# The attention of the first 256 tokens rebuilt, value matmuls with 64-column weights, and three weight groups split by VectorE and GpSimd

## The chip, the cores and the metric

One core of one Trainium2 chip runs the kernel. The metric is the device time of one execution in microseconds (us), as the median of several runs. TensorE does the matmuls, VectorE (DVE), ScalarE (ACT) and GpSimd (POOL) the element-wise work, and SyncE (SP) issues every transfer.

## The reference, cut to what matters

An attention with a window and sinks over 2 sequences of 768 tokens, 8 heads of 64, followed by two dense layers on the 1536 tokens (512 features in, 2048 inside, 512 out), all in float32:

```python
scores = scale * np.matmul(q, k.transpose(0, 1, 3, 2))
is_sink = pos[None, :] < n_sink                 # n_sink = 4
in_window = (rel >= 0) & (rel < window)         # window = 128
scores = np.where(is_sink | in_window, scores, -1e9)
a = softmax(scores)                             # max, exp, sum + 1e-9, divide
x = np.matmul(a, v)                             # heads side by side: 512 features
h = x @ w_in;  g = 0, h or (h + 1)**2 / 4       # first layer, by h <= -1, h >= 1, between
x = g @ w_out
h = x @ w_in2; g = h if h > 0 else exp(h) - 1   # second layer
y = g @ w_out2
```

## The kernel before, in words

Tokens are taken in six chunks of 256 (`NC = 6`). Activations lie with features on the partitions. For each chunk the attention gives `x` (4 tiles of 128 features, one for each pair of heads), and the first layer runs 16 steps `t` over the 2048 inner features: `hidden` (L457) makes 128 of them in 12 matmuls, `outward` (L474) adds the part of step `t-2` to the output in 12 more. The second layer runs over chunks of 512 tokens.

Precision: the layers' matmuls take operands in a rounded 32-bit form (fp32r), and each product is made of three matmuls (high by high, low by high, high by low), so every operand is split into a high part (a rounding copy on ACT) and a low part (source minus high on DVE). Weights come in 32 groups of 128x1024 (16 of each layer), through raw buffers, and are split once (`split_weights`, L581 on ACT, L757 on DVE).

The attention of chunk `c+1` is interleaved with the first layer of chunk `c` (the plan `BESIDE`); the attention of chunk 0 has nothing beside it and runs alone in front (`ALONE`). For one head: `split_head` (q and k into parts), `scores` (four fp32r matmuls of 260 columns, L414 and L415: 256 keys of the window and 4 sinks, for each of two blocks of 128 queries), `maxima` (a fused mask, scale and maximum in DVE, L716), `exponent` (ACT, L544), `normalise` (DVE, L724 to L730), `transposes` (TensorE, L426), the copy of the transposed probabilities (ACT, L550). For a pair of heads: `values`, whose weights have 128 columns of which 64 are zeros for either head (`vs` is 3*HD wide with zeros in it), so that both heads add into one bank of 128 partitions; these are plain float32 matmuls, each of which the trace shows as two records (L447 to L449), and one matmul for the sinks (L454). `write_x` and `split_x` then make `x`, `x_hi`, `x_lo`.

In chunk 0 the same steps run head by head with doubled buffers (banks of the layers, corners of `xy` and `wout_*`). Five weight groups (`EARLY = 5`, plan `SPLITS_ALONE`) are split by ACT and DVE inside this stretch; the other 11 of the first layer are split in chunk 0's layer, group `5+t` at step `t`. The layers start when `x_lo` of the first pairs and groups 0 and 1 are there. GpSimd only builds masks and copies the mask of each chunk (L402). SP issues all loads in one written-out order, waiting in it for buffers.

The order on every engine is written out by hand; engines meet only at semaphores.

Of the kernel before, what the change touches and what calls it, by code (L numbers as in the profile page):

```python
# [54 lines left out]
SPLITS_ALONE = {6: [0], 7: [1], 8: [2], 9: [3, 4]}  # L55
EARLY = sum(map(len, SPLITS_ALONE.values()))

# [3 lines left out]
def attention_plan(head_at, by_halves):  # L61

    scores, exps, transposes, values = ([[] for _ in range(head_at[-1] + 4)] for _ in range(4))
    for h, at in enumerate(head_at):
        scores[at].append(h)
        exps[at + 1].append(h)
        transposes[at + 2].append(h)  # L70
        if by_halves and h < HEADS - 2:
            values[at + 4].append((h // 2, [h % 2]))
        elif h % 2 == 1:
            values[at + 3].append((h // 2, [0, 1]))
    return scores, exps, transposes, values


ALONE = attention_plan(list(range(HEADS)), True)
BESIDE = attention_plan([2, 3, 5, 6, 8, 9, 11, 12], False)


def build(nc, q_t, k_t, v_w, v_s, w_in, w_out, ident_d, out, n_sink, window):
# [8 lines left out]
    with ExitStack() as ctx:  # L91
# [16 lines left out]
        small = sb("small", [P, 4 * QB + 1])  # L108
        top, total = (small[:, n:n + 2 * QB].rearrange("p (h j) -> p h j", h=2) for n in (0, 2 * QB))
        half = small[:, 4 * QB:4 * QB + 1]  # L110
# [14 lines left out]
        vs = sb0("vs", [P, 2, 3, 3 * HD])  # L125
        vsink = sb0("vsink", [P, 2, P])
# [19 lines left out]
        waited_act, waited_dve = sem("waited_act"), sem("waited_dve")  # L146
        qk_loaded = [sem(f"qk_loaded{n}") for n in range(4)]
# [33 lines left out]
        def tiles(parts, first, count, width):  # L181
            return parts[:, first:first + count, :].rearrange("p f m -> p (f m)")[:, 0:width]

        heads_at_once = [(k_hi[:, :], k_lo[:, :], q_parts[:, :], s_ps, t_ps),
                         (tiles(wout_hi, FT - 2, 2, QB * SW), tiles(wout_lo, FT - 2, 2, QB * SW),
                          tiles(wout_hi, FT - 3, 1, CT), h_ps, y_ps[0])]
        pairs_at_once = [(probs[:, :, :], (probs_t[:, 0, :], probs_t[:, 1, :]), xy[:, 2, 0:CT], o_ps),
                         (xy[:, 3, CT:CT + QB * 2 * SW].rearrange("p (j n) -> p j n", j=QB),
                          tuple(b[:, :, :].rearrange("p s t -> p (s t)") for b in (ramp, g_full)),
                          xy[:, 0, CT:2 * CT], y_ps[1])]  # L190
        pair_beside = (*pairs_at_once[0][:2], sinks_t[:, :], o_ps)
        loaded_heads = [(ks[:, s, :], qs[:, s, :]) for s in range(2)]
        loaded_heads += [(xy[:, 2, CT + s * QB * SW:CT + (s + 1) * QB * SW], q)
                         for s, q in enumerate((xy[:, 1, CT:2 * CT], xy[:, 3, 0:CT]))]

        def is_first(c):
            return isinstance(c, int) and c == 0

        assert CT + 2 * QB * SW <= TOK and QB * SW <= 2 * DM

        def head_work(c, h):

            return heads_at_once[h % 2 if is_first(c) else 0]

        def pair_work(c, p):


            return pairs_at_once[p % 2] if is_first(c) else pair_beside

        def loaded_head(c, h):  # L210
            return loaded_heads[h % 4 if is_first(c) else h % 2]

        def heads_before(c, h):
            return h - 1 if is_first(c) else c * HEADS + h

        def pairs_before(c, p):
            return p - 1 if is_first(c) else c * PAIRS + p
# [10 lines left out]
        FEW = RAW - 2  # L230
# [45 lines left out]

        block = ctx.enter_context(nc.Block())
# [3 lines left out]
        def _(sp):  # L281
            def load_head(c, h):

                if not is_first(c):
                    sp.wait_ge(qk_lo_ready, c * HEADS + (h - 1))
                elif h >= 4:
                    sp.wait_ge(qk_lo_ready, h - 3)
                for to, src in zip(loaded_head(c, h), (k_t, q_t)):
                    sp.dma_start(to, src[bass.ds(c * HEADS + h, 1)].rearrange("o p n -> (o p) n")).then_inc(qk_loaded[h % 4], 16)

            def load_values(c, p):
                s = p % 2
                if not is_first(c) or p >= 2:
                    sp.wait_ge(attn_ready, c * PAIRS + (p - 1))
                n = c * PAIRS + p
# [9 lines left out]
            def load_weights(i):  # L305
                n = order[i]
                layer, m = n // NW, n % NW
                if splits_until_free(i) > 0:
                    sp.wait_ge(w_lo_ready, splits_until_free(i))
                if i < NW and place[i] >= FEW:  # L310
                    sp.wait_ge(x_written, PAIRS)
                if i >= NW:
                    sp.wait_ge(attn_ready, NC * PAIRS)
# [3 lines left out]
            load_head(0, 0)  # L317
            load_head(0, 1)
            load_head(0, 2)
            sp.dma_start(ident[:, :], ident_d).then_inc(ident_loaded, 16)  # L320
            load_head(0, 3)
            load_head(0, 4)
            load_values(0, 0)
            load_weights(0)
            load_head(0, 5)
            load_head(0, 6)
# [566 lines left out]
```

## Time and profile before

| | |
|---|---|
| median of 3 runs | 666.1 us (665.94 to 667.99) |
| the profiled execution | 667.29 us, its span 665.3 us |
| TensorE matmuls busy | 642.4 us, 97% of the span |
| DVE, ACT, GpSimd busy | 390.8, 361.6, 9.4 us |
| first matmul of the layers | at 38.69 us of the span |
| second layer starts | at about 399 us |

The span runs from the first to the last instruction. The profiled execution took 2.0 us more than its span and 1.2 us more than the median of the runs.

### The profile page before, as it was taken

What the parts mean: (1) busy time and instruction counts of PE and PEld (TensorE: products, weight loads), DVE (VectorE), ACT (ScalarE), POOL (GpSimd) and SP (SyncE); (2) the same over time, 40 slices, a digit from 0 to 9 for tenths busy, and PEclk for the clock granted to TensorE, in tenths of its full rate; (3) what the DMA queues carried; (4) which work ended last, traced back from release to release, by engine and by line L of the source; (5) the groups of instructions that cost most, each with busy time, mean ns of one, the idle gap of its engine ahead of it and who ended that gap; (6) DMA issues with size and microseconds to landing.
All of it is one profiled execution on the core that took longest, in us unless ns stands there. A gap on an engine that the chain in (4) does not pass through costs nothing.

```text
span 665.3 us, 12399 instructions
## 1 busy us (share of the span) xinstructions
PE 642.4 (97%) x4204; PEld 582.4 (88%) x4204; DVE 390.8 (59%) x1022; ACT 361.6 (54%) x854; POOL 9.4 (1%) x28
## 2 busy tenths in 40 slices
PE   3888999999999999999999999999999999999998
PEld 3778999999999999999999998888888888888886
DVE  6989986886788588868866884322332222322221
ACT  6887766665665565656656665333453333533333
POOL 3000000000000000000000000000000000000000
PEclk9999999999999999999999999999999999999999
DMA  8477320431233023204205530000010000100001
GB/s 276 155 253 276 95 70 25 113 87 51 68 92 96 25 82 109 71 24 112 68 0 191 191 127 1 1 0 1 1 63 0 0 0 0 63 0 0 0 0 64
DMA packets 25805, 47.39 MB, mean 71 GB/s; under 512 B 2929, under 2 KB 10929, under 8 KB 25777
## 3 DMA queue, kind: packets, MB, share of 16 engines
q1 hardware_dynamic: 25776, 47.03, 22.7%
q8 instruction: 16, 0.26, 0.2%
q14 instruction: 13, 0.10, 0.0%
HBM read 43.88 MB, written 3.15 MB: 71 GB/s over the span
## 4 chain that ended last, share of the span: by engine, by line
PE 85%; DVE 11%; issue 2%; ACT 1%; DMA 1%; SPq 0%; ACTq 0%; DVEq 0%
PE h_ps L469 12%; PE h_ps L471 12%; PE h_ps L470 12%; PE y_ps L484 9%; PE y_ps L486 9%; PE y_ps L485 9%; PE s_ps L486 3%; PE s_ps L485 3%; PE s_ps L484 3%; PE o_ps L447 2%; PE t_ps L426 2%; PE s_ps L414 1%; DVE wout_lo L762 1%; PE s_ps L415 1%; PE o_ps L449 1%
## 5 line engine op out<-in xcount | busy, mean ns | idle before, releaser
L469 PE MATMUL h_ps<-x_hi,win_hi 128*128 128x256 f32 (+1 forms) x576 | 184.5, 320 | 1.3 <-DVE x_lo L769 0.5
L471 PE MATMUL h_ps<-x_hi,win_lo 128*128 128x256 f32 (+1 forms) x576 | 182.7, 317 | 0.0
L470 PE MATMUL h_ps<-x_lo,win_hi 128*128 128x256 f32 (+1 forms) x576 | 182.3, 316 | 0.0
L484 PE MATMUL y_ps<-g_hi,wout_hi 128*128 128x256 f32 (+1 forms) x480 | 145.2, 302 | 1.5 <-DVE g_lo L775 1.3
L486 PE MATMUL y_ps<-g_hi,wout_lo 128*128 128x256 f32 (+1 forms) x480 | 144.9, 302 | 0.0
L485 PE MATMUL y_ps<-g_lo,wout_hi 128*128 128x256 f32 (+1 forms) x480 | 144.6, 301 | 0.0
L792 DVE SCALAR_TENSOR_TENSOR g_full<-g_full,h_ps 128x512 f32<-128x512 f32 x48 | 33.0, 688 | 151.8 <-ACT g_full L622 151.8
L469 PEld LDWEIGHTS h_ps<-x_hi,win_hi 128*128 128x128 f32 x576 | 108.1, 188 | 11.1 <-DVE g_full L788 1.1
L470 PEld LDWEIGHTS h_ps<-x_lo,win_hi 128*128 128x128 f32 x576 | 108.2, 188 | 8.4
L471 PEld LDWEIGHTS h_ps<-x_hi,win_lo 128*128 128x128 f32 x576 | 108.2, 188 | 7.2
L775 DVE TENSOR_TENSOR g_lo<-g_full,g_hi 128x256 fp32r<-128x256 f32 (+1 forms) x144 | 73.6, 511 | 53.5 <-ACT g_hi L609 52.9
L609 ACT CAST g_hi<-g_full 128x256 fp32r<-128x256 f32 (+1 forms) x144 | 68.5, 476 | 66.7 <-DVE g_full L792 34.1
L484 PEld LDWEIGHTS y_ps<-g_hi,wout_hi 128*128 128x128 f32 x480 | 90.1, 188 | 7.2 <-issue 1.7
L485 PEld LDWEIGHTS y_ps<-g_lo,wout_hi 128*128 128x128 f32 x480 | 90.1, 188 | 4.2
L486 PEld LDWEIGHTS y_ps<-g_hi,wout_lo 128*128 128x128 f32 x480 | 90.1, 188 | 3.6
L620 ACT ACTIVATE ramp<-h_ps 128x512 f32<-128x512 f32 x48 | 28.8, 599 | 117.4 <-PE h_ps L471 116.8
L544 ACT ACTIVATE probs<-s_ps,small 128x260 f32<-128x260 f32 x84 | 39.2, 470 | 22.9 <-DVE small L719 22.9
L617 ACT ACTIVATE ramp<-h_ps,small 128x256 f32<-128x256 f32 x96 | 45.5, 474 | 5.7 <-PE h_ps L471 5.5
L786 DVE SCALAR_TENSOR_TENSOR g_full<-ramp 128x256 f32<-128x256 f32 x96 | 40.3, 420 | 8.8 <-ACT ramp L617 8.7
L788 DVE TENSOR_TENSOR g_full<-g_full,h_ps 128x256 f32<-128x256 f32 x96 | 40.4, 421 | 3.3
L550 ACT COPY probs_t<-t_ps 128x512 f32<-128x512 f32 x42 | 24.7, 588 | 24.8 <-PE t_ps L426 24.8
L486 PE MATMUL s_ps<-g_hi,wout_lo 128*128 128x512 f32 x96 | 37.8, 394 | 0.0
(122 smaller groups left out, 862.7 us busy)
## 6 DMA issues: line engine op xcount, KB each, us to landing
ks<-in_k SPq DMA_DIRECT2D x44, 260.0 KB, 2.7
vs<-in_v SPq DMA_DIRECT2D x24, 288.0 KB
qs<-in_q SPq DMA_DIRECT2D x44, 128.0 KB, 2.6
raw<-in_w_in SPq DMA_DIRECT2D x11, 512.0 KB, 4.6
raw<-in_w_out SPq DMA_DIRECT2D x11, 512.0 KB, 4.4
out_y<-xy SPq DMA_DIRECT2D x12, 256.0 KB, 2.1
xy<-in_w_in SPq DMA_DIRECT2D x5, 512.0 KB, 5.8
xy<-in_w_out SPq DMA_DIRECT2D x5, 512.0 KB, 6.3
```

What stands on the lines that cost most here:

```text
L469: pe.matmul(o, win_hi[:, k, f], x_hi[:, k, :], start=(k == 0), stop=False)
L470: pe.matmul(o, win_hi[:, k, f], x_lo[:, k, :], start=False, stop=False)
L471: last = pe.matmul(o, win_lo[:, k, f], x_hi[:, k, :], start=False, stop=(k == KT - 1))
L484: pe.matmul(o, wout_hi[:, t, cols], g_hi[:, t % GR, :], start=begin, stop=False, skip_group_check=True)
L485: pe.matmul(o, wout_hi[:, t, cols], g_lo[:, t % GR, :], start=False, stop=False, skip_group_check=True)
L486: last = pe.matmul(o, wout_lo[:, t, cols], g_hi[:, t % GR, :], start=False, stop=(t == FT - 1), skip_group_check=True)
L544: nc.scalar.activation(probs[:, j, hh * SW:(hh + 1) * SW], banks[j][:, 0:SW], ACT.Exp, bias=top[:, hh, j:j + 1], accum_out=total[:, hh, j: ...
L609: nc.scalar.copy(g_hi[:, t % GR, :], g_full[:, t % 2, :]).then_inc(g_hi_ready, 1)
L617: nc.scalar.activation(ramp[:, t % 2, :], h, ACT.Relu, bias=half[:, 0:1], scale=0.5).then_inc(ramp_ready, 1)
L775: nc.vector.tensor_tensor(g_lo[:, t % GR, :], g_full[:, t % 2, :], g_hi[:, t % GR, :].bitcast(F32), ALU.subtract).then_inc(g_lo_ready, 1)
L786: nc.vector.scalar_tensor_tensor(g, r, 1.0, r, ALU.min, ALU.mult).then_inc(bent_ready, 1)
L788: nc.vector.tensor_tensor(g, g, h, ALU.max).then_inc(g_ready, 1)
```

## The change

1. **The attention of chunk 0** is rewritten pair by pair, two pairs in flight. Query block 0 sees only its own 128 keys and block 1 sees 256 (`SEEN_OF`, 384 probabilities for a head instead of 520); sinks are inside the window there, so their columns, transposes and matmuls go. Scores are plain float32 matmuls on the 64 partitions of a head, with no split of q and k. Four maxima are followed by one negation for the pair, and one addition and one reciprocal serve four rows of sums. `x_hi` and `x_lo` are made from the bank (`x` itself is not written). q, k and v of the chunk have arrays of their own.
2. **The value matmuls of every chunk** take 64 weight columns and write the 64 partitions of their head; the two heads alternate. `vs` is 2*HD wide, without zeros.
3. **Three weight groups** (`EARLY = 3` instead of 5) are split ahead of the layers, by a copy on DVE and a subtraction on GpSimd; the remaining 13 are split at steps 0 to 12 of chunk 0 (`splits_first`). GpSimd's mask copy for chunk 1 stands behind its subtractions. `FEW` is 5 instead of 4, and the loads are issued in another order.

```diff
-SPLITS_ALONE = {6: [0], 7: [1], 8: [2], 9: [3, 4]}
-EARLY = sum(map(len, SPLITS_ALONE.values()))
+EARLY = 3
+SEEN = P + WIN
+SEEN_OF = (slice(0, P), slice(P, SEEN))
+KEYS_OF = (slice(0, P), slice(0, WIN))
+IN_FLIGHT = 2
-        FEW = RAW - 2
+        FEW = RAW - 1
...
# SyncE
+            load_first_head_pair(0)
+            load_first_head_pair(1)
+            sp.dma_start(ident[:, :], ident_d).then_inc(ident_loaded, 16)
+            load_first_values(0)
+            load_first_head_pair(2)
+            load_first_values(1)
+            load_weights(0)
+            load_first_head_pair(3)
+            load_first_values(2)
+            load_first_values(3)
+            load_weights(1)
             load_weights(2)
             load_weights(3)
             load_weights(4)
             load_head(1, 0)
+            load_head(1, 1)
+            load_values(1, 0)
             load_weights(5)
             load_weights(6)
+            load_head(1, 2)
             load_weights(7)
             load_weights(8)
             load_head(1, 3)
             load_values(1, 1)
+            load_weights(9)
...
# GpSimd
+            for i in range(EARLY):
+                hi, lo = w_parts(order[i])
+                pool.wait_ge(first_w_hi, i + 1)
+                nc.gpsimd.tensor_tensor(lo, split_source(i), hi.bitcast(F32), ALU.subtract).then_inc(first_w_lo, 1)
+            pool.wait_ge(first_max, HEADS * QB)
+            nc.gpsimd.tensor_copy(mask[:, :], masks[:, 1, :]).then_inc(mask_ready, 1)
...
# TensorE
+            def first_scores_of(p):
+                pe.wait_ge(first_qk_loaded[p], 32)
+                (q, k), banks = first_qk[p], flight[p % IN_FLIGHT][0]
+                if p >= IN_FLIGHT:
+                    pe.wait_ge(first_exp, (p - IN_FLIGHT + 1) * 2 * QB)
+                for j in range(QB):
+                    for hh in range(2):
+                        dims = slice(HD * hh, HD * (hh + 1))
+                        last = pe.matmul(banks[hh][:, SEEN_OF[j]], q[dims, j * P:(j + 1) * P], k[dims, KEYS_OF[j]], ...)
+                last.then_inc(first_scores, 1)
+            def first_transposes(p):
+                if p > 0:
+                    pe.wait_ge(first_copied, 2 * p)
+                for hh in range(2):
+                    pe.wait_ge(first_probs, (2 * p + hh + 1) * QB)
+                    for n in range(3):
+                        last = pe.transpose(h_ps[hh][:, n * P:(n + 1) * P], seen_probs(p, hh)[:, n * P:(n + 1) * P], ident[:, :])
+                    last.then_inc(first_probs_t, 1)
+            def first_values(p):
+                pe.wait_ge(first_v_loaded[p], 16)
+                pe.wait_ge(first_copied, 2 * (p + 1))
+                if p >= IN_FLIGHT:
+                    pe.wait_ge(x_lo_ready, p - IN_FLIGHT + 1)
+                for block, queries, keys_t in ((0, slice(0, CT), slice(0, CT)), (1, slice(P, CT), slice(CT, CT + P))):
+                    for hh in range(2):
+                        last = pe.matmul(o_bank[dims, queries], first_v[p][:, block * P + HD * hh:...], probs_t[hh][:, keys_t], ...)
+                last.then_inc(first_attn, 1)
...
-                for hh in halves:
-                    v, pt = vs[:, s, :, HD * hh:HD * hh + P], probs_t[hh]
-                    pe.matmul(o_bank[:, 0:CT], v[:, 1, :], pt[:, P:P + CT], ...)
-                    pe.matmul(o_bank[:, 0:P], v[:, 0, :], pt[:, 0:P], ...)
-                    pe.matmul(o_bank[:, P:CT], v[:, 2, :], pt[:, P + CT:P + CT + P], ...)
+                for block, queries, keys_t in ((1, slice(0, CT), slice(P, P + CT)), (0, slice(0, P), slice(0, P)),
+                                               (2, slice(P, CT), slice(P + CT, 2 * CT))):
+                    for hh in range(2):
+                        dims = slice(HD * hh, HD * (hh + 1))
+                        pe.matmul(o_ps[dims, queries], vs[:, s, block, dims], probs_t[:, hh, keys_t], ...)
...
+            first_scores_of(0)
+            first_scores_of(1)
+            first_scores_of(2)
+            pe.wait_ge(ident_loaded, 16)
+            first_transposes(0)
+            first_scores_of(3)
+            first_values(0)
+            for p in range(1, PAIRS):
+                first_transposes(p)
+                first_values(p)
...
# ScalarE: four exponents a pair, two copies of 384 columns a pair, one copy for x_hi
+            first_exponents(0)
+            first_exponents(1)
+            for p in range(PAIRS):
+                first_copies(p)
+                if p + IN_FLIGHT < PAIRS:
+                    first_exponents(p + IN_FLIGHT)
+                first_x(p)
...
# VectorE
+            def first_weights_hi(i):
+                dve.wait_ge(raw_loaded[place[i]], 16 * raw_count(i))
+                nc.vector.tensor_copy(w_parts(order[i])[0], split_source(i)).then_inc(first_w_hi, 1)
...
+            first_maxima(0)
+            first_maxima(1)
+            first_normalise(0)
+            first_maxima(2)
+            first_normalise(1)
+            first_maxima(3)
+            first_x(0)
+            first_normalise(2)
+            first_weights_hi(0)
+            first_x(1)
+            first_weights_hi(1)
+            first_normalise(3)
+            first_x(2)
+            first_weights_hi(2)
+            first_x(3)
```

`first_maxima`, `first_normalise` and `first_x` on DVE hold, for a pair: four fused maxima (128, 256, 128, 256 columns) and one negation; one addition, one reciprocal and four multiplications; one subtraction from the bank.

## Rows read from the trace of the kernel before

**Rows 1.** Page: the chain that ended last, by engine.
```profile
PE 85%; DVE 11%; issue 2%; ACT 1%; DMA 1%; SPq 0%; ACTq 0%; DVEq 0%
```
**Rows 2.** Windows by stage: us, busy of each engine, clock, DMA share, GB/s.
```profile
0.00:38.70 38.70, 25.50 (x129) 20.29 (x129) 30.10 (x97) 28.59 (x73) 6.89 (x24) 1.00 0.70 225
38.70:107.10 68.40, 63.23 (x511) 60.66 (x511) 60.62 (x163) 48.74 (x123) 0.63 (x1) 1.00 0.45 146
107.10:168.80 61.70, 61.37 (x514) 60.38 (x513) 47.52 (x149) 38.50 (x111) 0.63 (x1) 1.00 0.27 75
398.80:665.00 266.20, 263.23 (x1151) 215.63 (x1149) 74.84 (x108) 103.30 (x169) 0.00 (x0) 1.00 0.03 12
```
**Rows 3.** A window inside a later chunk of the first layer, same columns.
```profile
180.00:190.00 10.00, 10.00 (x85) 9.85 (x85) 8.82 (x28) 7.39 (x22) 0.00 (x0) 1.00 0.28 75
```
**Rows 4.** DVE in that chunk: start, us, then idle and its releaser.
```profile
192.63 0.17 DVE L724 TENSOR_SCALAR small<-small 128x2 f32<-128x2 f32 x1 [1.09 <-ACT probs L544]
```
**Rows 5.** The last chain in order of time: the front, and chunk 0.
```profile
2.14 3.93 DMA qs<-in_q
...
86.86 0.39 PE s_ps L414
```
**Rows 6.** TensorE in order of time, in front and at the layers' start.
```profile
18.06 1.13 PE L447 MATMUL o_ps<-probs_t,vs 128*128 128x256 f32 x2
18.98 0.64 PE L448 MATMUL o_ps<-probs_t,vs 128*128 128x128 f32 x2
...
21.24 0.59 PE L447 MATMUL o_ps<-probs_t,vs 128*128 128x256 f32 x2
21.67 0.38 PE L448 MATMUL o_ps<-probs_t,vs 128*128 128x128 f32 x2
...
22.20 0.69 PE L454 MATMUL o_ps<-xy,vsink 8*128 8x256 f32 x2
22.83 0.66 PE L426 MATMUL y_ps<-ident,xy 128*128 128x128 f32 x4
...
38.69 0.38 PE L469 MATMUL h_ps<-x_hi,win_hi 128*128 128x256 f32 x1
```
**Rows 7.** TensorE in order of time: one pair's values in a later chunk.
```profile
126.64 0.59 PE L447 MATMUL o_ps<-probs_t,vs 128*128 128x256 f32 x2
...
127.51 0.60 PE L447 MATMUL o_ps<-probs_t,vs 128*128 128x256 f32 x2
...
128.31 0.36 PE L454 MATMUL o_ps<-sinks_t,vsink_parts 72*128 72x256 f32 x1
```
**Rows 8.** TensorE and its weight loads (PEld) around transposes with 8 weight columns.
```profile
123.01 0.20 PEld L432 LDWEIGHTS o_ps<-ident,probs 128*8 128x8 f32 x2
...
123.11 0.38 PE L432 MATMUL o_ps<-ident,probs 128*8 128x128 f32 x2
123.22 0.19 PEld L414 LDWEIGHTS s_ps<-k_hi,q_parts 128*128 128x128 f32 x1
```
**Rows 9.** Groups with shapes kept apart: busy, mean ns, idle before, releaser.
```profile
L544 ACT ACTIVATE probs<-s_ps,small 128x260 f32<-128x260 f32 x84 | 39.2, 470 | 22.9 <-DVE small L719 22.9
...
L716 DVE CUSTOM_DVE_ANT_0 s_ps<-s_ps,mask 128x260 f32<-128x260 f32 x88 | 36.3, 450 | 0.8 <-PE s_ps L415 0.3
...
L730 DVE TENSOR_SCALAR probs<-probs,small 128x260 f32<-128x260 f32 x88 | 27.3, 353 | 1.5
...
L550 ACT COPY probs_t<-t_ps 128x512 f32<-128x512 f32 x42 | 24.7, 588 | 24.8 <-PE t_ps L426 24.8
...
L762 DVE TENSOR_TENSOR win_lo<-raw,win_hi 128x1024 fp32r<-128x1024 f32 x11 | 13.5, 1225 | 0.7 <-ACT win_hi L591 0.3
...
L769 DVE TENSOR_TENSOR x_lo<-xy,x_hi 128x256 fp32r<-128x256 f32 x24 | 8.8, 420 | 1.1 <-ACT x_hi L602 1.1
```
**Rows 10.** GpSimd's mask copy, and DVE while it ran.
```profile
30.97 0.62 POOL L402 COPY mask<-masks 128x528 bf16 x1 [22.06 <-DVE small L716]
...
31.19 0.55 DVE L730 TENSOR_SCALAR xy<-xy,small 128x260 f32<-128x260 f32 x1
```

More of the change, by code:

```diff
@@ L191, in build @@
[L191 to L203, printed above, removed]
@@ L392, in build_mask, with build_first_mask @@
                         step(nc.gpsimd.memset((own if j == 0 else prev)[:, 0:NS], MASKED / SCALE))
-            build_mask(mask[:, :], 0)
+            def build_first_mask(m):
+                step(nc.gpsimd.memset(m, 0.0))
+                own0, prev1, own1 = (m[:, n * P:(n + 1) * P] for n in range(3))
+                for own in (own0, own1):
+                    keep_where(own, 0, [[-1, P]], 1)
+                    if window < P:
+                        keep_where(own, window - 1, [[1, P]], -1)
+                keep_where(prev1, window - 1 - P, [[1, P]], -1)
+                for sinks in (own0, prev1):
+                    step(nc.gpsimd.memset(sinks[:, 0:NS], 0.0))
+            build_first_mask(mask[:, 0:SEEN])
             pool.sem_inc(mask_ready, 1)
@@ L496, in layer_chunk @@
                     if attend is not None:
-                        for p, halves in BESIDE[3][t]:
-                            values(attend, p, halves)
+                        for p in BESIDE[3][t]:
+                            values(attend, p)
                         for h in BESIDE[2][t]:
@@ L504, in layer_chunk @@
                 outward(layer, c, FT - 1)
-            for t in range(len(ALONE[0])):
-                for h in ALONE[0][t]:
-                    scores(0, h)
-                for p, halves in ALONE[3][t]:
-                    values(0, p, halves)
-                if t == 2:
-                    pe.wait_ge(ident_loaded, 16)
-                for h in ALONE[2][t]:
-                    transposes(0, h)
+            first_scores_of(0)
[8 more added lines that the diff above has]
+                first_values(p)
             layer_chunk(0, 0, 1)
@@ new lines, in first_copies, with first_x @@
+            def first_copies(p):
+                probs_t = flight[p % IN_FLIGHT][3]
+                if p >= IN_FLIGHT:
+                    act.wait_ge(first_attn, p - IN_FLIGHT + 1)
+                for hh in range(2):
+                    act.wait_ge(first_probs_t, 2 * p + hh + 1)
+                    nc.scalar.copy(probs_t[hh][:, 0:SEEN], h_ps[hh][:, 0:SEEN]).then_inc(first_copied, 1)
+            def first_x(p):
+                act.wait_ge(first_attn, p + 1)
+                nc.scalar.copy(x_hi[:, p, :], flight[p % IN_FLIGHT][1][:, 0:CT]).then_inc(x_hi_ready, 1)
```

363 lines of the change are left out of this document (181 added, 182 removed).

## The prediction

> **What bounds the kernel now.** I read the page's chain of waits first: TensorE carries 85% of the chain that ended last, DVE 11% [rows 1]. Then the windows by stage [rows 2], which show three regimes. In front, 38.70 us, no engine is full (DVE 30.10, ACT 28.59, TensorE 25.50 busy): a chain of latencies through three engines, with DVE the longest. The layer of chunk 0 takes 68.40 us, with DVE at 60.62. The chunk after it takes 61.70 us with TensorE at 61.37, and the three behind that are like it. The second layer, 266 us, isn't touched. The chain in order of time puts chunk 0's turn at 86.86 us: before it the chain runs through DVE, from there through TensorE [rows 5]. So time can be had in front, in TensorE's work of chunks 1 to 4 (those that have an attention beside them), and in DVE's of chunk 0 up to 86.86 us. A window inside a later chunk warns that DVE follows closely, 8.82 us of 10.00 [rows 3], and that some of its idle time is a latency that stays (1.09 us of waiting for the exponents, [rows 4]).
>
> **The value matmuls, pairs in chunks 1 to 4.** The values of a pair run from 126.64 to 128.31 = 1.67 us, of which one head takes 127.51-126.64 = 0.87 us [rows 7]. After the change there are as many float32 matmuls with the same columns. What can shrink is only their placing: the two heads use different halves of the weight columns and of the bank's partitions, and alternate. The bounds: nothing gained if the halves run one after another, and one head's 0.87 us if both run side by side throughout. No row shows two narrow matmuls side by side. The nearest row is that of the transposes with 8 weight columns: a load for 8 columns is issued at 123.01, before their first matmul at 123.11, and the load of the following 128-column matmul at 123.22, 0.11 us behind that first one, with no gap opened by the change of width [rows 8]. So narrow columns cost no emptying of the array there, and I take it that the halves do overlap. Each float32 matmul is two records one behind the other, and records start in order: of A1 A2 B1 B2 C1, B1 can start with A2, and C1 with B2 at the earliest. With 0.22 us for a record of 256 columns (21.67-21.24 = 0.43 for two) and 0.11 for 128, the twelve records end after 1.09 us instead of 1.74: 0.65 us a pair. I book 0.55, since entering and leaving may cost a little. 16 pairs lie in chunks 1 to 4: 8.8 us. In chunk 0 only the last pair lies behind 86.86 us: 0.5. Together 9.3 us. DVE covers none of it away as long as three steps with a pair beside them (72 matmuls of 0.118 us, that is 61.37/514 less a little, and about 3.8 us of attention: 12.3) stay longer than its work with its latency, 8.82/10 x 12.3 + about 0.7 = 11.5 us; 12.3-0.55 = 11.7 just does. That is the ceiling of this gain too.
>
> The Trainium skill, TensorEngine Tiling (Array Packing), sections Tiling Modes and Performance Considerations, says that column tiles of 64 run independently and up to 2x faster, but also that a change of tiling mode drains TensorE. No row here shows two tiles at once; on the drain, rows 8 speak against it for columns. By its first sentence the gain would be up to 0.87 us a pair, 14 us in all.
>
> A drain can be priced from a matmul with few rows. L448 and L449 end at 21.67 + 4 x 0.11 = 22.11; two records of L454 on 8 rows, 0.43 us of streaming, take until 22.83 [rows 6]. So 0.29 us go to entering and leaving, and another load of about 0.11 stands in front of the next matmul: 0.4 us a pair if columns behave as these rows did.
>
> **The front.** Removed: eight splits of q and k, sink transposes, copies and matmuls, a quarter of the softmax's columns, `x` itself, two weight groups on ACT and all five low parts on DVE. By rows 9, per pair on DVE: four maxima 2 x 0.45 + 2 x 0.31 (132 columns fewer, at (1225-420)/768 = 1.05 ns for a column) + 0.17 = 1.7 us; sums, reciprocals, four multiplications of 0.35 and less = 1.5; `x_lo` 0.42. Four pairs 14.5 us, and three copies of 128x1024. Those copies aren't in the trace: at most the 1.22 us of the subtraction of that size, at least half; I take 0.8. DVE: 17 us, against 30.10 busy before.
>
> The order on each engine, followed through: q and k of the first pair are there when ACT's first input was, 3.9 us. The scores in float32 on two half arrays, TensorE at its slow rate (L447 to L448 takes 0.92 us for two records at 18.06, 0.43 at 21.24: 1.2 and then 2.4 GHz, though the clock column says 1.00, [rows 6]): 384 columns for each of two heads, 2.6 us one by one and 1.3 side by side, and the load and entry; 3.0 taken, ready 6.9. Maxima 8.6, second pair's 11.6; exponents (four of 0.47 and 0.36 spaced) 10.4 and 13.3; normalised 13.1; scores of pair 2 ready 11.7; maxima of pair 2 14.8; normalise 1 16.3; maxima 3 18.0; `x` 0 18.4; normalise 2 19.9 (its exponents stood behind the first copies on ACT, 16.6); weight copy 0 20.8; `x` 1 21.4; then copy 1, normalise 3, and from there transposes 0.7, two copies of 384 columns 0.9, values 1.0. Without any clash this is 22.2, 23.7, 26.2 us for the layers' start.
>
> **GpSimd beside DVE.** What is to be feared is in [rows 10]: the mask copy ran from 30.97 to 31.59, and the multiplication that began at 31.19 took 0.55 us instead of 0.353 [rows 9]; it ended only behind it. GpSimd's subtraction of 128x1024 isn't in the trace. Its copy of 528 elements took 0.62 us, 1.2 ns for each; with one input 1.2 us for 1024, and with two float32 inputs I take twice that, 2.4, with 1.2 and 5 as bounds. Subtraction 0 runs 20.8 to 23.2 and holds copy 1 on DVE until then (24.0); subtraction 1, 24.0 to 26.4, holds the multiplications of pair 3 (27.5). Transposes, copies and values follow: the layers start at **30 us**, 8.7 earlier than 38.69. Bounds: 26.2 with no clash; 34 if TensorE stays slow in front or its half-array matmuls don't overlap. Subtraction 2, to about 30.5, is wanted at step 2, some 6 us later: hidden; at 5 us each it would not be.
>
> The Trainium skill, SBUF — State Buffer, section Who interferes with whom, has the rule: GpSimd and DVE share a pair of ports as an exclusive lock, for DVE copies in a two-port mode. Rows 10 agree with 0.2 us. The skill's GPSIMD Engine Reference, section Performance versus the Vector engine, gives 4497 ns for a two-input operation of 2048; as an estimate that is 2.25 us for 1024, and the sum would be the same within 0.5.
>
> **Chunk 0's layer.** Two more groups are split in it, at steps 11 and 12: 2 x 1.14 us on DVE, just where its binding ended at 86.86. Waits as in [rows 4], about 1 us, hide part: +1.2 us. Group 5's load waits for GpSimd, and the order in SP's queue is tighter: `load_head(1, 2)`, waiting for a split on DVE, stands in front of groups 7 and 8, and head 4's q and k stand behind group 15, whose buffer is free only after group 9's split at step 6, while head 4 is wanted at step 8. One step of about 4.3 us covers most of it: +0.5. Together +1.7, bounds 0 and 4. The narrower `vs` saves transfer in a stage with a DMA share of 0.27: nothing.
>
> **Sum.** Against the profiled execution: 667.3 - 8.7 - 9.3 + 1.7 = 651.0; less the 1.2 us by which it lies above the median, 649.8, so **650 us**.
>
> **Rivals.**
> - *The halves don't overlap* and cost nothing: 650 + 9.3 = 659. For it: no row shows an overlap, and a float32 matmul is two dependent records. Chance 0.22.
> - *They overlap, and entering and leaving costs 0.4 us a pair*: 0.25 left of 0.65, 4 us in all, 655. For it the 8-row matmul [rows 6], against it rows 8. This is the Trainium skill's sentence on changing the mode. Chance 0.16.
> - *TensorE stays at the slow rate in front* (gaps longer than its work), the halves overlap: start at 34, 654. It was at the fast rate from about 21 us, with less work in each gap. Chance 0.06.
> - *Slower*: narrow matmuls one by one, each waiting for its own load of 64 columns (0.055 us, half of the 0.11 that 128 columns take: loads and matmuls alternate at 61.70/514 = 0.12, [rows 2]), in all 12 x 0.055 + 0.4 = 1.05 us a pair, 16 pairs: 659 + 17 = 676. It turns the sign from 0.44 us a pair on. Against it: rows 8 show loads passing under narrow matmuls. Chance 0.04.
> - *My forecast*: halves overlap at little cost, start near 30. Chance 0.52; its own range is 641 (start at 26.2, 0.87 us a pair up to DVE's limit) to 654.
>
> **How the numbers follow.** A measurement tells from no change what is beyond about 0.3%, 2 us. Faster: all but the slow case, less a little for a long stall behind GpSimd: 0.94; same 0.02, slower 0.04. The range reaches from 641 to 661, the rivals below it in, the slower one and the tails of the front's bounds out.
>
> **What would show it.** Right: first layer matmul near 30 us; the value matmuls of a pair about 1.1 us apart from first to sinks, starts of both heads' records interleaved; chunks 1 to 4 near 59.5 us; chunk 0's layer near 70; GpSimd subtractions of 2 to 3 us, and one DVE copy or multiplication stretched by each. Wrong: 1.7 us or more a pair (no overlap); chunks that stay at 61.7 with TensorE waiting for DVE (DVE's limit sooner than I have it); 0.22 us a matmul far into chunk 0; GpSimd subtractions near 5 us, with step 0 or 2 waiting for them; ACT idle at step 8 on q and k.

## The result and the profile after

The changed kernel takes 662.41 us (median of 4 runs, 661.48 to 662.44) beside 666.02 us of the kernel before in the same series (4 runs, 665.91 to 667.99): the ratio is 0.9935, with a 95% interval of 0.9915 to 0.9956. It is faster by 3.6 us where 16 were forecast, and outside the range of 641 to 661. The profiled execution took 662.44 us, its span 660.7.

The windows by stage of the kernel after answer to [rows 2]: front, chunk 0's layer, the chunk behind it, the second layer (columns as there).

```profile
0.00:27.96 27.96, 16.55 (x89) 10.59 (x89) 17.47 (x68) 12.68 (x45) 12.23 (x25) 0.93 0.68 228
27.96:100.70 72.74, 65.38 (x513) 61.22 (x512) 62.27 (x163) 50.11 (x124) 2.16 (x3) 0.95 0.39 123
100.70:161.00 60.30, 60.07 (x510) 57.69 (x509) 47.06 (x149) 38.34 (x110) 0.63 (x1) 1.00 0.25 70
388.70:660.70 272.00, 268.65 (x1152) 215.80 (x1150) 75.32 (x109) 103.68 (x169) 0.00 (x0) 1.00 0.03 12
```

The front is 10.7 us shorter and the later chunks about 1 us each. But chunk 0's layer has grown by 4 us, and the second layer, in which no line was changed, has grown from 266 to 272 us. To put exact numbers on it I mark the stages by the first copy from a chunk's output banks, in both traces: before at 107.23, 168.53, 229.87, 291.20, 352.23 and 398.45 us; after at 100.75, 161.07, 221.40, 281.72, 341.74 and 388.67.

| stage | before | after | difference | forecast |
|---|---|---|---|---|
| front, to the layers' first matmul | 38.69 | 27.96 | -10.7 | -8.7 |
| from there to chunk 0's copy | 68.54 | 72.79 | +4.25 | +1.7 - 0.5 |
| chunks 1 to 4 | 245.00 | 240.99 | -4.0 | -8.8 |
| chunk 5 (no attention beside it) | 46.22 | 46.93 | +0.7 | 0 |
| second layer | 266.85 | 272.03 | +5.2 | 0 |
| span | 665.3 | 660.7 | -4.6 | -16.3 |

Did the value matmuls gain nothing? Here is TensorE in order of time around one pair's values, after; it answers to [rows 7].

```profile
120.37 0.27 PE L536 MATMUL y_ps<-g_hi,wout_lo 128*128 128x256 f32 x1
120.57 1.09 PE L503 MATMUL o_ps<-probs_t,vals 128*64 128x256 f32 x12
121.59 0.38 PE L505 MATMUL o_ps<-sinks_t,vsink_parts 72*128 72x256 f32 x1
121.81 0.28 PE L473 MATMUL s_ps<-k_hi,q_parts 128*128 128x260 f32 x1
```

From the first value matmul to the sinks: 121.59-120.57 = 1.02 us instead of 1.67, the 0.65 of the working, but not in its way. The line above merges twelve records; the same view, cut to 120.50 to 120.60, holds the first two of them:

```profile
120.57 0.44 PE L503 MATMUL o_ps<-probs_t,vals 128*64 128x256 f32 x2
```

Either record is 0.43 us long and both together 0.44, so the second head's first record starts with the first head's first one, and not, as the working had it, with its second. In front, where the rows keep the two heads apart, one sees the overlap itself: two 256-column records start 0.01 to 0.04 us apart, 0.24 us before the next two.

```profile
17.70 0.40 PE L463 MATMUL t_ps<-ramp,vals 128*64 128x256 f32 x1 [0.66 <-ACT g_full L594]
17.71 0.43 PE L463 MATMUL t_ps<-g_full,vals 128*64 128x256 f32 x1
17.94 0.38 PE L463 MATMUL t_ps<-ramp,vals 128*64 128x256 f32 x1
17.98 0.38 PE L463 MATMUL t_ps<-g_full,vals 128*64 128x256 f32 x1
```

The edges cost more than was booked. Around the same pair before, in rows that stand beside [rows 7], the last plain matmul began 0.12 us ahead of the values (now 0.20), and the scores 0.20 us behind the sinks' matmul (now 0.22).

```profile
126.52 0.28 PE L486 MATMUL y_ps<-g_hi,wout_lo 128*128 128x256 f32 x1
...
128.51 0.28 PE L414 MATMUL s_ps<-k_hi,q_parts 128*128 128x260 f32 x1
```

Inside the pair, record by record, the first one is followed by the second after 0.27 us (0.22 before), and the sinks' matmul begins 0.21 us behind the last value record (0.03 before). So the halves, side by side throughout, save one head's whole 0.87 us, and 0.08 + 0.05 + 0.18 + 0.02 = 0.33 us of it go to entering and leaving: 0.54 us a pair are left.

So the gain is there and something else takes it back. The groups with shapes kept apart, from 480 us on (inside the second layer), first before, then after:

```profile
L471 PE MATMUL h_ps<-x_hi,win_lo 128*128 128x512 f32 x128 | 50.4, 394 | 0.0
L470 PE MATMUL h_ps<-x_lo,win_hi 128*128 128x512 f32 x128 | 50.2, 392 | 0.0
L469 PE MATMUL h_ps<-x_hi,win_hi 128*128 128x512 f32 x128 | 49.7, 388 | 0.0
```
```profile
L521 PE MATMUL h_ps<-x_hi,win_lo 128*128 128x512 f32 x126 | 50.3, 399 | 0.0
L520 PE MATMUL h_ps<-x_lo,win_hi 128*128 128x512 f32 x126 | 49.6, 394 | 0.0
L519 PE MATMUL h_ps<-x_hi,win_hi 128*128 128x512 f32 x125 | 49.0, 392 | 0.0
```

Nothing waits (0.0 idle before), the granted clock is 1.00 in both, the instructions are the same, and the records are 2 to 5 ns longer. Records overlap, so the pace is told by the time from one start to the next: by product it is 226, 229 and 232 ns before, and 231, 232 and 237 ns after. On average that is 4.5 ns more, and 1152 x 4.5 ns = 5.2 us, the whole difference of the layer.

The other surprise is one stall in chunk 0. ACT's and DVE's first operation on head 4, and TensorE's first score, each with the idle time before it:

```profile
63.35 0.62 ACT L605 CAST k_hi<-ks 128x520 fp32r<-128x520 f32 x1 [3.03 <-DMA qs<-in_q]
64.31 0.70 DVE L795 TENSOR_TENSOR k_lo<-ks,k_hi 128x520 fp32r<-128x520 f32 x1 [2.74 <-ACT q_parts L606]
65.50 0.58 PE L473 MATMUL s_ps<-k_hi,q_parts 128*128 128x260 f32 x1 [3.42 <-DVE q_parts L796]
```

And GpSimd's subtractions with what DVE did meanwhile (two engines' rows, in order of time on each):

```profile
18.54 2.35 POOL L420 TENSOR_TENSOR win_lo<-raw,win_hi 128x1024 fp32r<-128x1024 f32 x1 [10.71 <-DVE win_hi L790]
21.52 2.34 POOL L420 TENSOR_TENSOR wout_lo<-raw,wout_hi 128x1024 fp32r<-128x1024 f32 x1 [0.63 <-DVE wout_hi L790]
25.68 2.35 POOL L420 TENSOR_TENSOR win_lo<-xy,win_hi 128x1024 fp32r<-128x1024 f32 x1 [1.81 <-DVE win_hi L790]
...
19.82 1.62 DVE L790 CAST wout_hi<-raw 128x1024 fp32r<-128x1024 f32 x1
...
21.77 2.90 DVE L781 TENSOR_SCALAR xy<-xy,small 128x128 f32<-128x128 f32 x4
...
24.92 0.68 DVE L790 CAST win_hi<-xy 128x1024 fp32r<-128x1024 f32 x1
```

The copy that began 1.28 us into a subtraction took 1.62 us instead of 0.68; the four multiplications took 2.90 instead of 1.01.

### The profile page after: what moved, and what is told of

It reads as the page before. It is cut to its first block, busy times and chain, and to the rows that moved or that the text cites. A ratio compares the mean times of both kernels' runs of the same rounds, so it can differ in the third digit from the quotient of the medians.

```text
span 660.7 us, 12095 instructions
## 1 busy us (share of the span) xinstructions
PE 637.7 (97%) x4164; PEld 564.7 (85%) x4164; DVE 379.7 (57%) x994; ACT 347.6 (53%) x827; POOL 16.3 (2%) x30
## 4 chain that ended last, share of the span: by engine, by line
PE 88%; DVE 7%; DMA 2%; issue 1%; ACT 1%; SPq 1%; ACTq 0%; DVEq 0%
PE h_ps L519 13%; PE h_ps L521 13%; PE h_ps L520 13%; PE y_ps L534 10%; PE y_ps L536 9%; PE y_ps L535 9%; PE s_ps L536 3%; PE s_ps L535 3%; PE s_ps L534 3%; PE o_ps L503 3%; PE t_ps L483 2%; PE s_ps L473 1%; PE s_ps L474 1%; DVE wout_lo L851 1%; DMA xy<-in_qk_first 1%
## 5 line engine op out<-in xcount | busy, mean ns | idle before, releaser
L519 PE MATMUL h_ps<-x_hi,win_hi 128*128 128x256 f32 (+1 forms) x576 | 187.5, 326 | 0.3
L521 PE MATMUL h_ps<-x_hi,win_lo 128*128 128x256 f32 (+1 forms) x576 | 185.7, 322 | 0.0
L520 PE MATMUL h_ps<-x_lo,win_hi 128*128 128x256 f32 (+1 forms) x576 | 184.8, 321 | 0.0
L534 PE MATMUL y_ps<-g_hi,wout_hi 128*128 128x256 f32 (+1 forms) x480 | 146.9, 306 | 1.4 <-DVE g_lo L864 1.4
L536 PE MATMUL y_ps<-g_hi,wout_lo 128*128 128x256 f32 (+1 forms) x480 | 146.4, 305 | 0.0
L519 PEld LDWEIGHTS h_ps<-x_hi,win_hi 128*128 128x128 f32 x576 | 109.4, 190 | 10.5 <-DVE g_full L877 1.0
L520 PEld LDWEIGHTS h_ps<-x_lo,win_hi 128*128 128x128 f32 x576 | 109.9, 191 | 9.4
L615 ACT ACTIVATE probs<-s_ps,small 128x260 f32<-128x260 f32 x80 | 37.4, 471 | 25.8 <-DVE small L811 25.7
L535 PE MATMUL s_ps<-g_lo,wout_hi 128*128 128x512 f32 x96 | 37.8, 394 | 0.0
```

What stands on the lines that cost most here:

```text
L519: pe.matmul(o, win_hi[:, k, f], x_hi[:, k, :], start=(k == 0), stop=False)
L520: pe.matmul(o, win_hi[:, k, f], x_lo[:, k, :], start=False, stop=False)
L521: last = pe.matmul(o, win_lo[:, k, f], x_hi[:, k, :], start=False, stop=(k == KT - 1))
L534: pe.matmul(o, wout_hi[:, t, cols], g_hi[:, t % GR, :], start=begin, stop=False, skip_group_check=True)
L535: pe.matmul(o, wout_hi[:, t, cols], g_lo[:, t % GR, :], start=False, stop=False, skip_group_check=True)
L536: last = pe.matmul(o, wout_lo[:, t, cols], g_hi[:, t % GR, :], start=False, stop=(t == FT - 1), skip_group_check=True)
```

## The experiments

Where could a slower matmul come from that nobody edited? One thing did move: the small tensor of maxima and sums grew from 9 to 17 floats for a partition. Tensors are placed one behind the other at multiples of 32 bytes, and the weight parts lie in front of it, every activation that the layers multiply behind it. The other tensors up to these activations have a multiple of 256 bytes, so before, activations lay 64 bytes (modulo 256) from the weights, after the change 96. The table below and the word distance mean this number. The first theory was narrower, that a start at a multiple of 64 bytes is enough; rivals were the new form of the value matmuls, and the chip itself.

**1. The small tensor at 48 floats (distance 192).**

```diff
-        small = sb("small", [P, IN_FLIGHT * 4 * QB + 1])
+        small = sb("small", [P, 48])
```

> The changed kernel with one edit: the small tensor of row maxima and sums is declared 48 floats wide instead of 17, so that all tensors allocated behind it start at a multiple of 64 bytes again (17 floats put them 32 bytes beyond one). Theory A (the start address of the moving operands sets the pace of all matmuls): 512-column matmuls go back from 0.2335 us apart to 0.229, 256-column ones from 0.120 to 0.118, the second layer from 272 to 267 us, the chunks of the first layer with attention from 60.3 to about 58.7, the whole to about 650. Rival B (the pace comes from something else that the new program does, its code or its clock): no change, 662.

Measured: 651.42 us (650.74 to 652.02), ratio to the kernel before 0.9774 [0.9758, 0.9791]. One number in one line gives 11 us, 9 of them in the first layer and 1.6 in a front whose code is the same (26.40 us instead of 27.96). Chunks of 58.39 us instead of 60.32; but the second layer stays at 271.98 where 267 was expected. So the place matters, and not in the same way for both layers.

**2. The kernel before, with only the 64-column values.** `vs` 2*HD wide, values as in the diff of the change, part 2; `small` untouched (distance 64).

> The kernel before with one part of the change alone: value matmuls with 64 weight columns, the two heads alternating, in all chunks (vs 2*HD wide). Nothing in the addresses changes. If the two halves of the array overlap as in the changed kernel's trace (a pair from first value matmul to the next attention matmul 1.24 us instead of 1.87), chunks 1 to 4 take 61.3 - 4 x 0.63 = 58.8 us each, and the whole 666 - 10 - up to 1 in chunk 0 = about 656. Rival (DVE is the next limit and takes the gain back): chunks stay above 60.

Measured: 659.64 us (658.62 to 660.04), ratio 0.9896 [0.9878, 0.9914]. Chunks 1 to 4 go from 61.33 to 59.55, 1.78 us for four pairs, 0.45 a pair where 0.63 was expected; the second layer keeps its 266.84.

**3. The same, and the small tensor of 17 floats (distance 96).**

```diff
-        small = sb("small", [P, 4 * QB + 1])
+        small = sb("small", [P, 17])
```

> The kernel before with narrow value matmuls, and in addition the small tensor 17 floats wide instead of 9, as the change has it, so that the tensors behind it start 32 bytes beyond a multiple of 64. Theory A: the second layer goes from 267 to 272 us and the whole is 12 us slower than with narrow values alone, about 668. Rival B: same as with narrow values alone.

Measured: 668.33 us (667.75 to 668.75), ratio 1.0032 [1.0019, 1.0045]. 8.7 us slower than run 2 for eight unused floats: chunks 60.32, chunk 5 46.92, second layer 271.94, the changed kernel's numbers. With it the whole gain of the values is gone.

**4. Run 1, with head 4's q and k ahead of groups 14 and 15.**

```diff
-            for i in range(10, NW):
-                load_weights(i)
-            load_pair(1, 2)
+            for i in range(10, 14):
+                load_weights(i)
+            load_head(1, 4)
+            load_weights(14)
+            load_weights(15)
+            load_head(1, 5)
+            load_values(1, 2)
```

> The changed kernel with aligned tensors and another load order: q and k of head 4 of chunk 1 in front of weight groups 14 and 15, those of head 5 behind group 15. In the changed kernel ACT waited 3.0 us for head 4's q at step 8 of chunk 0, and TensorE 3.4 us for the split behind it. Theory: the loads stood behind group 15's wait for a buffer, the wait goes, and 2 to 3.4 us are gained over the aligned kernel, about 647. Rival: the DVE is full in chunk 0 and the stall was hidden in it: under 1 us.

Measured: 648.92 us (648.27 to 650.58), ratio 0.9748 [0.9728, 0.9769]. Chunk 0 from its first matmul to its copy: 69.44 us instead of 72.43, the stall's 3.0 us. The medians differ by 2.5.

**5. Run 4, with GpSimd's three subtractions on DVE.** The copies of groups 1 and 2 stand behind the last normalisation.

```diff
-            for i in range(EARLY):
-                hi, lo = w_parts(order[i])
-                pool.wait_ge(first_w_hi, i + 1)
-                nc.gpsimd.tensor_tensor(lo, split_source(i), hi.bitcast(F32), ALU.subtract).then_inc(first_w_lo, 1)
...
-                nc.vector.tensor_copy(w_parts(order[i])[0], split_source(i)).then_inc(first_w_hi, 1)
+                hi, lo = w_parts(order[i])
+                nc.vector.tensor_copy(hi, split_source(i)).then_inc(first_w_hi, 1)
+                dve.wait_ge(first_w_hi, i + 1)
+                nc.vector.tensor_tensor(lo, split_source(i), hi.bitcast(F32), ALU.subtract).then_inc(first_w_lo, 1)
...
-            first_weights_hi(1)
             first_normalise(3)
             first_x(2)
+            first_weights_hi(1)
             first_weights_hi(2)
```

> This is the aligned kernel with head 4's loads early (648.9 us), with the subtraction of the three early weight groups taken from GpSimd and given to VectorE, groups 1 and 2 behind the third normalisation. Theory that GpSimd's subtractions hold VectorE's casts and copies (the front's VectorE operations of 0.69 us took 1.62, a group of 1.01 took 2.90, and TensorE waited 3.2 us behind it): no stretched VectorE operation in the front, the layers start at about 24.5 to 25.5 us instead of 26.7, total 646 to 648 us. Rival, that the start is set by the loads of the groups and not by the held VectorE: start within 0.3 us of 26.7, total 648.5 to 650 us. Second rival, that the subtractions (about 1 us each) now stand in VectorE's own way: start at 27.5 to 29, total 650 to 652 us.

Measured: 644.79 us (644.28 to 645.23), ratio 0.9681 [0.9665, 0.9697]. The layers start at 22.30 us instead of 26.74, earlier than any of the three expectations had it. DVE in order of time:

```profile
19.14 1.01 DVE L781 TENSOR_SCALAR xy<-xy,small 128x128 f32<-128x128 f32 x4
20.06 0.42 DVE L785 TENSOR_TENSOR x_lo<-o_ps,x_hi 128x256 fp32r<-128x256 f32 x1
20.40 0.68 DVE L791 CAST wout_hi<-raw 128x1024 fp32r<-128x1024 f32 x1
21.11 1.22 DVE L793 TENSOR_TENSOR wout_lo<-raw,wout_hi 128x1024 fp32r<-128x1024 f32 x1
```

Neither the multiplications nor the copy is stretched (2.90 and 2.80 us in run 4), and a subtraction takes 1.22 us here, 2.35 on GpSimd. TensorE's transposes of the last pair, first in run 4, then in run 5:

```profile
23.14 1.51 PE L454 MATMUL h_ps<-ident,xy 128*128 128x128 f32 x6 [4.40 <-DVE xy L785]
```
```profile
19.84 0.91 PE L450 MATMUL h_ps<-ident,xy 128*128 128x128 f32 x6 [1.09 <-DVE xy L781]
```

From there to the layers' first matmul it is 3.60 us in run 4, at a granted clock of 0.50 behind an idle time of 4.40 us, and 2.46 us in run 5, at 0.95. So of the 4.4 us some 1.1 lie in this stretch, beside the change of the clock. The run also moved the last normalisation in front of copy 1, so the other 3.3 us are GpSimd's hold on DVE and the order together; how they divide wasn't tried.

**6 to 8. Run 4 with other distances.** Only the width of `small` differs: 32, 64 and 80 floats, distances of 128, 256 and 320 bytes.

> The kernel of 648.9 us with the small tensor 32 floats wide: everything behind it starts 128 bytes behind the base, instead of 192. Theory A, that only the remainder by 64 bytes counts for the first layer: chunks of 58.4 us as at 192. Theory B, that each start address has a pace of its own by its remainder by 128 or 256: chunks unlike 58.4, between 58 and 60.5 us. Second layer: 266.9 us if it wants an address that 96 and 192 are not, 272 if it is fast at 64 alone.

> The same with 64 floats: 256 bytes behind the base. By theory A chunks of 58.4 us again; by theory B and a period of 128 bytes the same times as at 128; by a period of 256 those of an address that is a multiple of 256, which no run has had yet. Second layer 266.9 or 272 us, and it tells the same way.

> The same with 80 floats: 320 bytes behind the base, which is 64 more than a multiple of 256, as in the kernel before. If the pace goes by the remainder by 128 or 256 bytes: second layer 266.9 us again and the chunks of the first 59.5 us as in the narrow version of the kernel before; total about 650 us. If the absolute place counts (the distance to the weights, not the remainder): second layer other than 266.9 us.

Measured, one run each: 654.65, 649.52 and 648.83 us. By stage, with the runs above:

| distance (modulo 256) | kernels | chunk 1 | second layer | 512-column records, ns, sorted |
|---|---|---|---|---|
| 64 | run 2 | 59.55 | 266.84 | 394, 392, 388 |
| 64 (320) | run 8, run 12 | 59.51, 59.55 | 266.8 | 394, 392, 388 |
| 96 | after, run 3 | 60.32 | 272.0 | 399, 394, 392 |
| 128 | run 6 | 59.94 | 270.9 | 395 |
| 192 | runs 1, 4, 5 | 58.4 to 58.6 | 272.0 | 396 |
| 0 (256) | run 7 | 60.17 | 264.3 | 389 |

Theory A (the remainder by 64 alone) falls in the first layer: 128 and 256 give 59.9 and 60.2, not 58.4. Nor is the second layer at 266.9 or 272 there, as expected, but at 270.9 and 264.3. In these two columns every distance has a time of its own, 320 repeats 64 to the ns, and 64 and 192 differ: a period of 256 bytes fits every run, one of 128 doesn't. And where the first layer's chunks are fastest, at 192, the second layer is as slow as at 96. The distances 128 and 0 (in the first layer) stand on one kernel each. Chunk 5, with no attention beside it, doesn't follow its distance (last section).

**9. Each layer at its own best distance.** Run 5, with 64 bytes of padding in front of the second layer's own tensors, so that the first layer keeps 192 and the second has 0.

```diff
         first_layer.close()
+        pad1 = sb("pad1", [P, 16])
```

> The kernel of 644.8 us (first layer's tensors 192 bytes behind the base, its chunks at 58.4 us) with 16 floats of padding in front of the second layer's own tensors, so that they start at a multiple of 256 bytes, where the second layer took 263.8 us from the last copy instead of 271.5. If each layer's pace goes by its own tensors' start address: 644.8 - 7.7 = 637 us (636 to 638.5), 512-column records of 389 ns. If both layers' pace hangs on something else that the padding of the whole had moved: 644 to 645.5 us.

Measured: 637.01 us (636.43 to 638.25), ratio 0.9548 [0.9531, 0.9566]. Windows of its chunk 1 and its second layer:

```profile
92.22:150.70 58.48, 58.10 (x511) 55.76 (x510) 46.66 (x149) 38.10 (x110) 0.63 (x1) 1.00 0.26 72
370.68:635.00 264.32, 261.02 (x1152) 215.80 (x1150) 75.20 (x109) 103.63 (x169) 0.00 (x0) 1.00 0.03 12
```

Each layer keeps the time of its own distance, and this is the fastest version: 30 us under the kernel before.

**10. Run 9 with the values head by head in the later chunks.**

```diff
-                for block, queries, keys_t in ((1, slice(0, CT), slice(P, P + CT)), (0, slice(0, P), slice(0, P)),
-                                               (2, slice(P, CT), slice(P + CT, 2 * CT))):
-                    for hh in range(2):
+                for hh in range(2):
+                    for block, queries, keys_t in ((1, slice(0, CT), slice(P, P + CT)), (0, slice(0, P), slice(0, P)),
+                                                   (2, slice(P, CT), slice(P + CT, 2 * CT))):
```

> The kernel of e9 with the values' matmuls of a pair in the later chunks ordered head by head (three of the one, then three of the other) instead of alternating; same instructions, same operands. If two 64-column matmuls overlap only when the neighbours in the queue lie on different column halves: a pair takes about 1.5 to 1.7 us instead of 1.02, in 16 pairs 8 to 10.5 us more than e9. If the narrower matmul is cheap by itself, or the halves run apart in any order: less than 2 us more.

Measured: 646.28 us, one run. TensorE in order of time, around a pair:

```profile
111.98 0.28 PE L537 MATMUL y_ps<-g_hi,wout_lo 128*128 128x256 f32 x1
112.18 1.57 PE L504 MATMUL o_ps<-probs_t,vals 128*64 128x256 f32 x12
113.68 0.39 PE L506 MATMUL o_ps<-sinks_t,vsink_parts 72*128 72x256 f32 x1
```

1.50 us a pair instead of 1.02: most of the overlap comes from the alternating order, not from narrow weights as such. Some is left. Record by record, the second head's first matmul starts 0.49 us behind the first head's, beside the first head's second matmul (0.48) and ahead of the first head's third (0.70), though that one stands in front of it in the program. From chunk 0's copy to chunk 4's it costs 242.33-233.61 = 8.7 us, 0.54 for each of 16 pairs.

**11. Run 5 with the weights moved as well, by 128 bytes.** Activations then start 320 bytes behind the old base, their distance from the weights stays 192.

```diff
+        pad0 = sb("pad0", [P, 32])
         win_hi, win_lo = sb("win_hi", [P, KT, DFF], F32R), sb("win_lo", [P, KT, DFF], F32R)
```

> The kernel of 644.8 us with 32 floats of padding in front of the weights, so that weights and activations move together by 128 bytes: the activations then start 320 bytes behind the old base (64 more than a multiple of 256), and their distance from the weights stays what it was. If the address of the activations alone sets the pace: the pattern of an offset of 64 or 320, 512-column records of 394, 392 and 388 ns and a second layer of 266.4 us. If the distance to the weights sets it: 396, 396 and 395 ns, 271.5 us and chunks of 58.4 us, total unchanged within 0.5 us.

Measured: 646.99 us, one run; its layers started 3.1 us later than in run 5. The stages decide:

```profile
94.81:153.29 58.48, 58.10 (x511) 55.77 (x510) 46.65 (x149) 38.06 (x111) 0.63 (x1) 1.00 0.26 72
373.22:645.20 271.98, 268.68 (x1152) 216.52 (x1150) 75.23 (x109) 103.65 (x169) 0.00 (x0) 1.00 0.03 12
```

58.48 and 271.98 us are the times of a distance of 192, not the 59.5 and 266.8 of an address of 320. So, by this one shift, it is the distance between weights and activations that counts, not where the activations lie. All weight parts have the same remainder, and the next matmul's weights are loaded while one runs (as in [rows 8]), so the runs don't tell whether its own weights or the next ones count. The total was expected within 0.5 us of run 5's and is 2.2 us above it; why it started later, with the same front, is in the last section.

**12. The changed kernel at the distance of the kernel before.** Nothing altered but `small`, 80 floats.

```diff
-        small = sb("small", [P, IN_FLIGHT * 4 * QB + 1])
+        small = sb("small", [P, 80])
```

> The changed kernel with nothing altered but the width of the small tensor, 80 floats instead of 17: the activations' distance from the weights is then, by its remainder at 256 bytes, that of the kernel before (64). If the shift by 32 bytes is what the prediction lacked: chunks of 59.5 us instead of 60.3, the last without attention 46.2 instead of 46.9, a second layer of 266.8 instead of 272.0 us, so that 662.4 - 5.2 - 4 x 0.8 - 0.7 - 0.5 (the first chunk's share) = 652.8 us (651.5 to 654). If something else of the change had slowed the plain matmuls: 659 us or more.

Measured: 651.95 us (650.6 to 652.98), ratio 0.9776 [0.9758, 0.9794].

```profile
99.55:159.10 59.55, 59.28 (x511) 56.89 (x510) 46.94 (x149) 38.37 (x110) 0.63 (x1) 1.00 0.25 71
382.36:649.20 266.84, 263.56 (x1152) 215.92 (x1150) 75.23 (x109) 103.52 (x169) 0.00 (x0) 1.00 0.03 12
```

This is the change as the prediction thought of it, and it is 10.5 us faster than the change as it was made. Between the two profiled spans lie 11.5 us: 8.3 in chunks 1 to 4 and the second layer, 2.0 in chunk 5 (of which the distance explains 0.7), 0.9 in the front and 0.3 in chunk 0.

## Why the prediction was wrong

- **The step that failed is the first part's "the second layer, 266 us, isn't touched", and with it a sum that had no term for what every matmul costs.** Not a line of that layer was edited, but its operands were moved: 32 bytes between weights and activations. At the profile's spans this cost 5.2 us in the second layer, 0.77 in each of chunks 1 to 4 (60.32-59.55, runs 3 and 2) and 0.7 in chunk 5, 9.0 us in all, and some tenths in chunk 0. Runs 3 and 12 show it from both sides, +8.7 and -10.5 us. None of the rivals had it either, so neither the range nor the chances could.
- **Without the shift the sum holds.** Run 12 took 651.95 us against 650 forecast, its span 649.2 against 665.3-16.3 = 649.0. But that is luck in part, since errors cancel in it. Front -11.7 us (forecast -8.7), chunk 0 +4.0 (+1.2), chunks 1 to 4 -7.1 (-8.8), chunk 5 -1.3 (0, and no row shows why).
- **Value matmuls: the halves overlap, as forecast, but two terms were off and cancelled.** The working let the second head start with the first head's second record, 0.65 us, and booked 0.1 for entering and leaving. The rows have both heads start together, 0.87 us, and entering and leaving take 0.33. By the rows a pair thus gains 0.54 us, beside 0.55 booked, and that is luck; by the chunks of run 2 it is 0.45, 7.1 us in all beside 8.8, a quarter less. Most of the last 0.1 us a pair lies in the layer's own 256-column matmuls: in run 2 they start about 1 ns further apart than before (118 instead of 117 ns), 0.3 to 0.4 us in the 384 of a chunk. Why, no run shows. The Trainium skill, TensorEngine Tiling (Array Packing), section Tiling Modes, has column tiles work at the same time and a drain at a change of mode: the rows agree with the first, and bound the second at 0.33 us a pair. The rival's price of 0.4 was thus nearer than the 0.1 booked; it falls by its result, 0.25 us a pair, because the overlap is larger than either had.
- **Front: right in kind, 2 us too timid.** 27.96 us against 30, with the same code at 26.40 to 27.03 in runs 1, 4 and 12. Subtraction 0 began at 18.54, not 20.8; it takes 2.35 us, as the 2.4 of the working had it, and each of the first two stretched one piece of DVE's work, as forecast. The Trainium skill, SBUF — State Buffer, section Who interferes with whom, tells of this lock, and the trace agrees: the copy ended 0.55 us behind the first subtraction, the multiplications 0.8 us behind the second. TensorE's slow rate in front, a rival in the working, did occur in part: six transposes took 1.54 us at 10.46, 0.87 at 18.51, and 1.51 again at 24.35, behind 3.18 us of waiting for the stretched multiplications. The granted clock is 1.00 until 24 us and about 0.5 from there to 30, and the first matmuls of the layers stand 0.2 us apart until about 31 us. The front ended early all the same.
- **Chunk 0: the size of one term was off.** Booked were 0.5 us for head 4's q and k behind group 15; it was a stall of 3.0 to 3.4 us (rows above), and run 4 gives back 3.0. The working compared the step at which the buffer comes free with the step at which the head is wanted, and left out the way between: the load of the last weight group issued at 58.31 us, then k's and q's at 58.70 and 59.18, then 4.15 us until q landed (2.6 is the median of q's loads on the page). The DMA share of 0.27 that the working gave this stage is the next chunk's; this one's was 0.45 [rows 2]. Behind the stall the granted clock was 0.50 from 66 to 68 us. The other 1.2 us for two more splits is about right: with the stall gone chunk 0 takes 69.44 us (run 4) against 68.54, 0.9 more.
- **DVE's ceiling** in the later chunks wasn't met: run 9's chunks take 58.48 us, TensorE busy 58.10.

## What to carry to other kernels

Where one engine does thousands of equal instructions, compare their pace before and after first, also in stages that weren't edited: 2 to 5 ns in 400 took back 9 us of this change, which was left with 3.6. A buffer that grows moves all tensors behind it, so keep the distance between the weights and what they multiply fixed (here modulo 256 bytes), and try a few paddings, one for each layer: by the stages two paddings gave 9 and 8 us (runs 1 and 9), together more than the attention rebuilt in front (10.7). And where two halves of an array work side by side, alternate them in the queue and price the way in and out. Price a load from the moment its buffer is free through issue and landing, not by the step that frees it.

## What of the hardware was not expected

- A matmul's pace depends on the distance between weights and activations in SBUF, modulo 256 bytes: records of 512 columns take 389 ns at 0, 395 at 128, 396 at 192, 388 to 394 at 64, 392 to 399 at 96. From start to start that is 229 ns at 0, 232 at 64, 235 at 128 and 236 at 96 and 192 (the second layer's time by 1152). A first layer's chunk with its attention takes 58.4 us at 192 and 60.3 at 96. Why, the runs don't show: moving and stationary operands being read at once is my guess, and it wasn't tried with other sizes.
- The distance isn't all. Chunk 5's 256-column matmuls have two paces at one distance: 46.2 us for the chunk in run 8 and 44.9 in run 12 (both 64), 46.1 in run 1 and 44.9 in runs 4, 5, 9 (all 192). From start to start that is 118 and 113 ns, through nearly the whole chunk. These kernels differ in the order of a few loads, but not consistently, and each has the trace of one execution only. It stays open.
- TensorE's granted clock in front differs between kernels with the same front. The windows of its first 22 us, in run 11 and in run 9:

```profile
0.00:22.00 22.00, 14.25 (x75) 9.14 (x76) 14.17 (x66) 11.87 (x43) 5.85 (x23) 0.74 0.68 230
```
```profile
0.00:22.00 22.00, 12.97 (x84) 8.92 (x86) 15.86 (x69) 12.48 (x45) 5.85 (x23) 1.00 0.77 246
```

At a mean of 0.74 between the two levels (1.2 and 2.4 GHz) the front of run 11 got through fewer instructions and the layers started at 25.39 us; at 1.00 they started at 22.44 in run 9. These are one execution each, and the clock is the difference that the trace shows: some 3 us of a front made of short matmuls with gaps go with it, which is as much as an edit may bring. Compare starts only beside this column.
